# A fused attention, mixture-of-experts and MLP kernel: where three engines choose the expert program

## What is computed

```python
# attention, per step t
y[:, :, t] = einsum('bhd,bhde->bhe', rt, state + einsum('bhd,bhe->bhde', u * kt, vt))
state = w * state + einsum('bhd,bhe->bhde', kt, vt)
# experts: N, D, E, F = 1536, 384, 8, 1024; capacity 384
expert_idx = argmax(x @ w_gate, axis=1)          # a token keeps its place if
disp[e, counts[e]] = x[i]                        # counts[e] < capacity
h = maximum(einsum('ecd,edf->ecf', disp, w1), 0)
y = einsum('ecf,efd->ecd', h, w2)
out[i] = gate_w[i] * y[expert_idx[i], pos[i]]
# MLP: d_ff 2048
out = maximum(x @ w_in, 0) ** 2 @ w_out
```

## Time and profile before

| | us |
|---|---|
| three timed runs | 459.97, 468.36, 467.12 |
| median | 467.12 |
| profiled execution | 460.31 |
| its span, first to last instruction | 458.5 |
| TensorE matmul busy | 424.7 (93%) |
| VectorE busy | 287.2 (63%) |
| ScalarE busy | 212.2 (46%) |
| GpSimd busy | 103.0 (22%) |

### The profile page before, as it was taken

The page is one execution under the profiler, slowest core; times in us unless marked ns, Lnnn a source line. Parts: engine busy times, 40 slices in busy tenths (PEclk is TensorE's granted clock), DMA queues, the critical chain, the costliest instruction groups (busy, mean ns, idle before and its releaser), DMA issues.

```text
span 458.5 us, 8058 instructions
## 1 busy us (share of the span) xinstructions
PE 424.7 (93%) x2922; PEld 399.2 (87%) x2922; DVE 287.2 (63%) x490; ACT 212.2 (46%) x371; POOL 103.0 (22%) x102
## 2 busy tenths in 40 slices
PE   3999789764999999999999999999999999999993
PEld 2999779743999999999999889899899898898993
DVE  8888899852578776766864755455553554554431
ACT  3456455221455655665663643544444445444321
POOL 6897788039201101100000000001200002100003
PEclk9999999957999999999999999999999999999998
DMA  7999984016696556655556223232332242300001
GB/s 204 242 300 326 333 251 159 18 44 242 211 316 233 173 200 232 208 180 192 202 185 206 93 83 125 69 108 100 137 132 74 69 137 97 110 0 0 2 0 69
DMA packets 20475, 69.46 MB, mean 151 GB/s; under 512 B 2840, under 2 KB 9257, under 8 KB 20448
## 3 DMA queue, kind: packets, MB, share of 16 engines
q1 hardware_dynamic: 18656, 64.40, 43.6%
q0 software_dynamic: 1792, 4.72, 2.9%
HBM read 62.82 MB, written 7.08 MB: 152 GB/s over the span
## 4 chain that ended last, share of the span: by engine, by line
PE 81%; DVE 11%; issue 4%; DMA 1%; POOL 1%; ACT 0%; DVEq 0%; POOLq 0%; ACTq 0%
PE bank L505 34%; PE bank L528 22%; PE bank L518 13%; PE bank L470 4%; PE bank L452 3%; DVE wlo L813 2%; PE bank L468 2%; DVE am L831 1%; PE bank L460 1%; PE bank L446 1%; PE bank L495 1%; DVE ru L835 1%; DMA xg<-attention_out,gidx 1%; DVE St L848 1%; DVE cv L838 0%
## 5 line engine op out<-in xcount | busy, mean ns | idle before, releaser
L813 DVE TENSOR_TENSOR wlo<-raw,whi 128x1536 fp32r<-128x1536 f32 (+1 forms) x60 | 102.8, 1714 | 91.8 <-ACT whi L641 88.2
L641 ACT ACTIVATE whi<-raw 128x1536 fp32r<-128x1536 f32 x56 | 83.3, 1489 | 83.2 <-PE bank L528 47.6
L422 POOL DMA_INDIRECT out<-osb,oidx x12 | 13.0, 1081 | 247.9 <-ACT osb L755 245.4
L528 PE MATMUL bank<-whi,hhi 128*128 128x384 f32 x192 | 64.9, 338 | 0.5 <-DVE hlo L967 0.5
L528 PE MATMUL bank<-wlo,hhi 128*128 128x384 f32 x192 | 64.9, 338 | 0.0
L528 PE MATMUL bank<-whi,hlo 128*128 128x384 f32 x192 | 64.8, 338 | 0.0
L505 PE MATMUL bank<-xshi,whi 128*128 128x240 f32 x192 | 53.9, 281 | 6.3 <-issue 6.3
L505 PE MATMUL bank<-yhi,whi 128*128 (+1 forms) x144 | 56.9, 395 | 0.0
L505 PE MATMUL bank<-yhi,wlo 128*128 (+1 forms) x144 | 56.8, 395 | 0.0
L505 PE MATMUL bank<-ylo,whi 128*128 (+1 forms) x144 | 56.8, 395 | 0.0
L698 ACT ACTIVATE rl<-bank 128x512 f32<-128x512 f32 x48 | 28.6, 600 | 54.5 <-PE bank L505 51.0
(11 more groups left out here) (158 smaller groups left out, 782.6 us busy)
## 6 DMA issues: line engine op xcount, KB each, us to landing
raw<-in_wts SPq DMA_DIRECT2D x56, 768.0 KB, 4.3
feat<-in_feat SPq DMA_DIRECT2D x12, 448.0 KB, 10.6
rk<-in_rk SPq DMA_DIRECT2D x12, 384.0 KB, 8.2
vx<-in_vx SPq DMA_DIRECT2D x12, 224.0 KB, 11.5
vT<-in_vT SPq DMA_DIRECT2D x12, 192.0 KB, 10.0
attention_out<-x_sb SPq DMA_DIRECT2D x12, 192.0 KB, 8.5
out<-rl SPq DMA_DIRECT2D x12, 192.0 KB
xg<-attention_out,gidx POOLq DMA_INDIRECT x16, 4.0
```

What stands on the lines that cost most here:

```text
L422: nc.gpsimd.indirect_dma_start(out=out[:, :], out_offset=bass.IndirectOffsetOnAxis(ap=oidx[:, t:t + 1], axis=0), in_=osb[:, t, :], in_offs ...
L528: mm = pe.matmul(ps_o[tt][:, 0:DM], x[:, par, ft, tt * P:(tt + 1) * P], w[:, r, cols], start=(v == 0 and ft == 0 and step == 0), stop=(v = ...
L641: return nc.scalar.activation(dst, src, ACT.Copy)
L813: lo = v.tensor_tensor(wlo[:, r, at], raw[:, r, at], whi[:, r, at].bitcast(F32), ALU.subtract)
```

## The change

In TensorE's, ScalarE's and VectorE's streams the work on the first expert's rows moves from ahead of `by_peak` into the function that `by_peak` calls, so that it stands in both programs, behind the jump. TensorE now waits for `count_ready` directly after the routing's last matmul, where it waited for `gidx_ready` before; that wait goes. VectorE's `gates()` (four small operations) and `split_lo(2, 2)` move too. GpSimd's and SyncE's streams stay as they are.

```diff
--- before.py
+++ after.py
@@ -543,16 +543,6 @@
                 for _ in range(count):
                     pe.matmul(ps_tr[:, 0:E * CT * NT], ones_b[:, :], match[:, :, :].rearrange("p t s -> p (t s)"), start=True, stop=True)
 
-            pe.wait_ge(gidx_ready, 1)
-            warm(18)
-            for q in range(2):
-                pe.wait_ge(first_gathered[q], 16)
-                for k in range(KT):
-                    mm = pe.transpose(ps_e[k][:, q * P:(q + 1) * P], xg[0][:, q, k * P:(k + 1) * P], ident[:, :])
-                    if q == 1:
-                        mm.then_inc(xt_psum, 1)
-            warm(6)
-            pe.wait_ge(count_ready, 1)
 
             def expert_pair(i, last, x):
                 for j in range(2):
@@ -595,7 +585,18 @@
                 pe.wait_ge(w_lo, MOE_UNITS + 1)
                 hidden(0, ps_h[0], *compact(0), CHUNK)
 
+            def first_rows():
+                warm(18)
+                for q in range(2):
+                    pe.wait_ge(first_gathered[q], 16)
+                    for k in range(KT):
+                        mm = pe.transpose(ps_e[k][:, q * P:(q + 1) * P], xg[0][:, q, k * P:(k + 1) * P], ident[:, :])
+                        if q == 1:
+                            mm.then_inc(xt_psum, 1)
+                warm(6)
+
             def moe(x):
+                first_rows()
                 if x.tiles > 2:
                     pe.wait_ge(first_gathered[2], 16)
                     pe.wait_ge(xs_ready, KT)
@@ -609,6 +610,7 @@
                     expert_pair(i, False, x)
                 expert_pair(E // 2 - 1, True, x)
 
+            pe.wait_ge(count_ready, 1)
             by_peak(pe, moe)
             for t in range(NT):
                 pe.wait_ge(onehot, NT + t + 1)
@@ -699,11 +701,6 @@
                 for ft in range(2):
                     act.wait_ge(h_relu, 2 * (m - MOE_UNITS) + ft + 1)
                     nc.scalar.activation(hhi[:, par, ft, :], rl[:, ft, :], ACT.Square).then_inc(h_hi, 1)
-
-            for k in range(KT):
-                act.wait_ge(xt_psum, k + 1)
-                copy(xshi[0][:, k, 0:PAIR], ps_e[k][:, 0:PAIR]).then_inc(xs_hi, 1)
-            act.wait_ge(count_ready, 1)
 
             def expert_pair(i, last, x):
                 for j in range(2):
@@ -726,9 +723,13 @@
                     if not final:
                         split_hi(4 * e + EQ + 3, 3, e + 2)
 
+            act.wait_ge(count_ready, 1)
             act.wait_ge(starti_ready, 1)
 
             def moe(x):
+                for k in range(KT):
+                    act.wait_ge(xt_psum, k + 1)
+                    copy(xshi[0][:, k, 0:PAIR], ps_e[k][:, 0:PAIR]).then_inc(xs_hi, 1)
                 if x.tiles > 2:
                     act.wait_ge(xt_psum, x.first)
                     copy(xshi[0][:, :, PAIR:CAP], ps_tr[:, 0:KT * P].rearrange("p (k n) -> p k n", n=P)).then_inc(xs_hi, 1)
@@ -966,16 +967,6 @@
                     dve.wait_ge(h_hi, 2 * m + ft + 1)
                     v.tensor_tensor(hlo[:, par, ft, :], sq[:, ft, :], hhi[:, par, ft, :].bitcast(F32), ALU.subtract).then_inc(h_ready, 1)
 
-            gates()
-            for k in range(KT):
-                dve.wait_ge(xs_hi, k + 1)
-                v.tensor_tensor(xslo[0][:, k, 0:PAIR], ps_e[k][:, 0:PAIR], xshi[0][:, k, 0:PAIR].bitcast(F32),
-                                ALU.subtract).then_inc(xs_ready, 1)
-            dve.wait_ge(count_ready, 1)
-            dve.wait_ge(starti_ready, 1)
-
-            split_lo(2, 2)
-
             def expert_pair(i, last, x, between=None):
                 for j in range(2):
                     e, final = 2 * i + j, last and j == 1
@@ -1000,6 +991,12 @@
                         between[2 * j + 1]()
 
             def moe(x):
+                gates()
+                for k in range(KT):
+                    dve.wait_ge(xs_hi, k + 1)
+                    v.tensor_tensor(xslo[0][:, k, 0:PAIR], ps_e[k][:, 0:PAIR], xshi[0][:, k, 0:PAIR].bitcast(F32),
+                                    ALU.subtract).then_inc(xs_ready, 1)
+                split_lo(2, 2)
                 if x.tiles > 2:
                     dve.wait_ge(xs_hi, x.first)
                     v.tensor_tensor(xslo[0][:, :, PAIR:CAP], ps_tr[:, 0:KT * P].rearrange("p (k n) -> p k n", n=P),
```

## The result

The changed kernel took 467.54 us (median of 20 runs, 461.70 to 472.63), the kernel before 464.42 us (20 runs, 459.05 to 470.09). The ratio of the two is **1.0061, with a 95% interval from 1.0033 to 1.0088**: slower by some 3 us, where I forecast 456.0 us (452.5 to 466) and a gain of 4.3 us. Measured again as e9, the changed kernel gave 0.9993 [0.9948, 1.0039]: that it is slower is not certain, but a gain of 4.3 us (0.9907) lies outside both intervals.

The account below looks back on a forecast made before the run. TensorE was taken to be bound by waiting for the code it jumps to; about 1.9 us from an earlier start and 2.4 from the clock gave 460.31 − 4.3 = 456.0 us, range 452.5 to 466.

Parts of the forecast that it names:

- The bound: TensorE's 6.3 us idle ahead of the first `hidden`: it waits for the code its branch jumps to, 6,499 ns.
- Step 1: TensorE's register load and branch go ahead: the branch starts at 99.4 us, 0.9 us after `peaki` is written.
- Step 2: TensorE's code fetch at the earlier branch, on a nearly empty DMA, takes 3.5 us instead of 6.5.
- X: Price of the code fetch at TensorE's branch: 3.5 us taken, bounds 45 ns and 6.5 us.
- Rival A: At TensorE's branch the fetch still costs 6.5 us: gain only 1.3 us, 459.0 us; chance 0.26.
- rival B: TensorE's branch is nearly free once the DMA is quiet: gain 6.6 us, limited by gathers, 453.7 us; chance 0.10.
- Step 3: TensorE's work behind the branch: `warm(18)` for 4.3 us, then transposes; `hidden` can start at 109.0 us, not 111.18.
- Step 5: ScalarE's and VectorE's earlier branches: fetch of 3.5 us or less, `gates()` 0.8 us, hidden under over 3 us of cover.
- step 6: Queues: GpSimd's stream unchanged and TensorE's `gidx_ready` wait gone, each 0; the 4.3 us stay to the end.
- Step 4: TensorE's clock: the first two `hidden` run at full clock, 4.0 instead of 6.43 us, ending 4.3 us sooner.
- The sum: Whole kernel: 460.31 − 4.3 = 456.0 us, about 1.9 from the earlier start and 2.4 from the clock.
- Rival C: Full clock comes only behind the first two `hidden`; with a 6.5 us fetch, 1.2 us slower, 461.5 us; chance 0.10.

Follow-up runs that it names:

- e9: The changed kernel measured and profiled again, nothing altered; ratio to the kernel before 0.9993 [0.9948, 1.0039].
- e8: e1 with the narrow program directly behind the branch, the jump over the wide one at the experts' end; ratio to the kernel before 0.9930 [0.9892, 0.9967].
- e1: The changed kernel, but VectorE's `gates()` stay ahead of its branch, as before the change; ratio to the kernel before 0.9886 [0.9849, 0.9922].

## Why the prediction was wrong

**The bound, right.** TensorE waits for the code that it jumps to. e8 shows it: 71 ns without a far jump, 5,509 ns at the place to which the jump moved.

**Step 1, right.** TensorE's branch starts 0.9 us after `peaki`, as forecast.

**Step 2, right.** X was taken as 1.0 + 1.0 + 1.5 = 3.5 us; it is 1.0 + 1.3 + 1.4 = 3.7, and 3.34 to 3.92 in the other versions with an early branch. Rival A (6.5 us) and rival B (under 1 us) fall. What was to hold B to a gain of 6.6 us, gathers' packets until 12.5 us after `peaki`, did not hold: e8 reaches the second expert's transposes after 11.6 us and does not wait for a gather there.

The Trainium skill's page "Advanced Engine Details and Errata", section "Control Flow Timing", has about 108 ns for a compare-and-branch, as cited with B. e8's 71 ns, where the target follows, come near it; a far jump does not.

**Step 3, right up to the transposes.** `warm(18)` starts at 4.7 us (4.6 forecast), the transposes at 9.0 us (8.9). `hidden` was to start at 10.5 us and starts at 15.0.

**Step 5, wrong: this is the failing step.** It said that VectorE, after its own fetch of code, runs `gates()` in 0.8 us under a cover of over 3 us. The fetch was close: first work 3.8 us behind its branch, 5.5 us after `peaki` (3.5 and 5.0 forecast). But `gates()` took from 113.37 to 122.22 us, 8.9 us. I took its duration from a place where GpSimd clears nothing. I had asked of the moved operations only what they wait for by semaphores, and step 6 put GpSimd at nothing because its stream does not change; what it does beside VectorE's new place was never looked at. The `tensor_scalar` takes 8.09 − 0.17 = 7.9 us too long, and `hidden` starts 15.0 − 10.7 = 4.3 us later than in e1: the cover took 3.6 us of it, about what step 5 had counted on, and it was not enough.

The Trainium skill's page "SBUF — State Buffer", section "Who interferes with whom", says that VectorE's second port pair is GpSimd's only one, locked for a whole instruction; a `tensor_scalar` in a two-port mode takes it, a `tensor_tensor` with both inputs in SBUF competes only with a GpSimd operation that reads. The traces agree: 8.09, 8.12 and 0.84 us for the `tensor_scalar` beside memsets, 0.17 for the `tensor_tensor`. By the same section the engine that issues first gets the pair. That order can't be read here: the record of the held `tensor_scalar` starts 0.24 us ahead of the memset's.

The timing was close, too. By step 5's own figures `gates()` would have run from 5.0 to 5.8 us after `peaki`, and the first memset starts 6.0 us after it. So this collision could have been named as a rival, and priced at up to two memsets, but step 5's times alone did not make it certain. Both profiles of the changed kernel show it; how many of the other executions have it is not shown.

**Step 4, right but for that wait.** With `hidden` directly behind the warm matmuls, e1's 36 matmuls take 112.84 − 108.74 = 4.1 us (4.0 forecast). In the changed kernel the 4.4 us of idle time cost the clock, and they take 128.55 − 122.82 = 5.7 us.

**The sum.** 4.3 us were forecast; e1 measures 19.1 − 14.8 = 4.3 us of stage and a ratio of 0.9886. The changed kernel gives back 4.3 us of wait and 1.6 us of clock, 5.9 in all: the stage is 1.6 us longer than before. Rival C, the one slower case, named the first two `hidden` and their clock, but for another cause: it needed a branch of over 5.3 us. I gave C 0.10 and had no rival in which another engine's work slows a moved operation.

## What to carry to other kernels

Before an operation is moved, look at what each other engine does at the new place, and not only at semaphores: on VectorE this `tensor_scalar`, beside a long write of GpSimd, waited until that write ended (8.09 us instead of 0.17), and so did everything queued behind it. Code that a far jump reaches cost TensorE 3.3 to 6.5 us here; a jump is best placed where other engines' work covers it, and filler matmuls behind it are worth their time only if the clock gives more back (18 of them cost 4.3 us and gave back 1.6).

## What the runs showed of the hardware

A `tensor_scalar` on 12 elements whose record starts 0.24 us ahead of GpSimd's memset was still held, and over two memsets in a row (8.09 us), without getting in between them. TensorE's branch with its fetch took 6.1 to 6.5 us beside the weight loads and 3.3 to 3.9 us where the DMA's share was under 0.3. On the same code ahead of it, two executions reached `peaki` 9.4 us apart; a change of 1% is read from a stage, not from the ends of two profiles.
